# Exponent operands built on ScalarE, weight halves in other pieces, and wider moving operands in the output products of a gated attention and expert kernel

## The reference

```python
B, H, S, D = 4, 8, 768, 40
for t in range(S):                        # stabilised gated linear attention
    m_new = max(f[t] + m, i[t])
    C = exp(f[t] + m - m_new) * C + exp(i[t] - m_new) * outer(v[t], k[t])
    n = exp(f[t] + m - m_new) * n + exp(i[t] - m_new) * k[t]
    y[t] = sigmoid(o[t]) * (C @ q[t]) / max(abs(n @ q[t]), 1)
x = y.transpose(0, 2, 1, 3).reshape(3072, 320)
x = top-1 of 8 experts: gate * (relu(x @ w1[e]) @ w2[e]),  w1 320x1024, w2 1024x320
x = soft mixture with 32 slots over 8 experts (a softmax over tokens in, one over slots out)
```

## Time and profile before

| | us |
|---|---|
| median of 3 runs | 586.22 |
| lowest and highest | 584.45 and 593.98 |
| the profiled execution | 585.13 |
| its span, first to last instruction | 583.3 |
| PE busy in the span | 507.0 (87%) |
| DVE / ACT / POOL busy | 326.4 / 193.9 / 327.0 |
| mean granted TensorE clock | 0.947 |

### The profile page before, as it was taken

One profiled execution on the slowest core, in us unless ns is written; L12 is line 12 of the kernel. 1 busy time (PEld: TensorE's weight loads), 2 busy tenths in 40 slices (PEclk: granted clock), 3 DMA queues, 4 the chain that ended last, 5 costly groups with the idle time before them and its releaser, 6 DMA issues.

```text
span 583.3 us, 11329 instructions
## 1 busy us (share of the span) xinstructions
PE 507.0 (87%) x3819; PEld 429.3 (74%) x3820; DVE 326.4 (56%) x547; ACT 193.9 (33%) x424; POOL 327.0 (56%) x301
## 2 busy tenths in 40 slices
PE   0599999999993379999999999999999999979583
PEld 0388888888782368989898889889889899863222
DVE  7446687876865927435856666664654333342113
ACT  2234644646632303232323232323232323220003
POOL 2466878778775056549994959592596332102000
PEclk9999999999976569999999999999999999988897
DMA  7026898888720033456232424240411740039947
GB/s 213 0 67 226 244 310 257 275 253 268 247 85 22 0 93 102 114 147 188 104 127 87 144 82 149 71 160 11 147 67 33 248 159 6 3 110 347 319 157 270
DMA packets 30239, 86.22 MB, mean 148 GB/s; under 512 B 4720, under 2 KB 15072, under 8 KB 28160
## 3 DMA queue, kind: packets, MB, share of 16 engines
q1 hardware_dynamic: 23408, 75.07, 40.2%
q0 software_dynamic: 2480, 5.59, 3.7%
q10 hardware_dynamic: 4320, 5.15, 2.5%
HBM read 72.67 MB, written 8.37 MB: 139 GB/s over the span
## 4 chain that ended last, share of the span: by engine, by line
PE 62%; DVE 17%; issue 8%; POOL 7%; DMA 3%; ACT 1%; SPq 0%; DVEq 0%; POOLq 0%; ACTq 0%
PE bank L1335 7%; PE bank L1337 6%; PE bank L1336 6%; PE bank L1318 5%; PE bank L1320 4%; PE bank L1319 4%; PE bank L1346 4%; PE bank L1211 4%; PE bank L1194 3%; DVE ys L884 3%; PE bank L1360 3%; DVE gates L1041 3%; POOL hb L531 2%; PE bank L1464 2%; PE bank L1322 2%
## 5 line engine op out<-in xcount | busy, mean ns | idle before, releaser
L1335 PE MATMUL bank<-W_high,h_high 128*128 x248 | 79.1, 319 | 2.0 <-DVE h_low L1066 2.0
L627 POOL TENSOR_TENSOR W_high<-W,ones 128x3072 fp32r<-128x3072 f32 (+1 forms) x12 | 58.6, 4884 | 38.7 <-PE bank L1337 38.7
L1337 PE MATMUL bank<-W_low,h_high 128*128 x248 | 76.4, 308 | 0.0
L1336 PE MATMUL bank<-W_high,h_low 128*128 x248 | 76.4, 308 | 0.0
L593 POOL TENSOR_TENSOR W_low<-W,W_high 128x3072 fp32r<-128x3072 f32 (+1 forms) x12 | 74.8, 6237 | 0.9
L777 ACT ACTIVATE h_high<-bank 128x512 fp32r<-128x512 f32 x62 | 33.7, 595 | 122.9 <-PE bank L1346 118.7
L875 DVE RECIPROCAL hb<-hb 128x320 f32<-128x320 f32 x24 | 51.7, 2153 | 27.7 <-POOL hb L531 27.7
L636 POOL DMA_INDIRECT combine_slots<-gates,back_i x31 | 29.8, 961 | 60.4 <-ACT gates L765 36.1
L1022 DVE TENSOR_TENSOR yc<-bank,slot_gate 128x320 f32<-128x320 f32 x31 | 15.2, 491 | 74.9 <-PE bank L1337 74.9
L1318 PE MATMUL bank<-W_high,x_high 128*128 x124 | 52.4, 422 | 4.9 <-DVE x_high L1049 2.5
L1041 DVE TENSOR_TENSOR gates<-gates,rmx (+1 forms) x31 | 53.0, 1712 | 0.0
(11 more groups left out here) (245 smaller groups left out, 1082.3 us busy)
## 6 DMA issues: line engine op xcount, KB each, us to landing
ys<-in_kvo_rows_dram SPq DMA_DIRECT2D x24, 484.0 KB, 5.6
ys<-in_qk_columns_dram SPq DMA_DIRECT2D x24, 448.0 KB, 4.4
W<-in_moe_w_rows_dram SPq DMA_DIRECT2D x8, 1280.0 KB, 9.0
W<-in_moe_w_main_dram SPq DMA_DIRECT2D x8, 1024.0 KB, 6.4
W<-in_moe_w_rows_dram SPq DMA_DIRECT2D x10, 640.0 KB, 9.9
W<-in_moe_w_main_dram SPq DMA_DIRECT2D x10, 512.0 KB, 5.7
xs<-ys ACTq DMA_DIRECT2D x29, 160.0 KB, 2.1
W<-in_moe_w_rest_dram SPq DMA_DIRECT2D x16, 256.0 KB, 6.5
```

Source lines behind the costliest of these rows:

```text
L627: g.tensor_tensor(W_high[:, columns(e % 2, part_)], w, ones[:, 0:1].broadcast_to(list(w.shape)), ALU.mult).then_inc(high_ready, 1)
L1335: mm(dst, h_high[:, kk, :], high, start=(kk == 0), stop=False)
L1336: mm(dst, h_low[:, kk, :], high, start=False, stop=False)
L1337: last = mm(dst, h_high[:, kk, :], w2_at(W_low, slot, kk), start=False, stop=(kk == NF - 1))
```

## The change

1. `expand_gates` leaves POOL and goes to ACT. Instead of one 64x1024 and one 64x512 product per chunk there are 8 + 4 scaled copies of 64x128, four of them at the end of each of ACT's iterations 4c, 4c + 1 and 4c + 2. The signal `exp_next` comes with the last of the third four.
2. POOL's `split_low_piece` starts at i = 23 instead of 20. Pieces 0, 1 and 2 come in iterations 23, 24 and 25, and pieces 3, 4 and 5 after the loop.
3. ACT's `high_piece` has 8 pieces of 768 and 640 columns instead of 5 of 1024 and 1280, in iterations 13 to 20 instead of 17 to 21.
4. In `outputs` a product streams up to three heads (123 columns) instead of two (82). The results that are kept are the same.

```diff
@@ gpsimd
-            def expand_gates(c):
-
-                if c >= 2:
-                    pool.wait_ge(e_done, B * (c - 1))
-                pool.wait_ge(w_ready, B * (c - 1) + 1)
-                ch.step(g.tensor_tensor(exp_rows[c % 2][0:HD], split_gates[0:HD, c * P:(c + 1) * P].unsqueeze(1).broadcast_to([HD, H, P]),
-                                        head_of[0:HD, :].unsqueeze(2).broadcast_to([HD, H, P]), ALU.mult))
-                g.tensor_tensor(exp_cols[c % 2][HD:P], split_gates[HD:P, c * P:(c + 1) * P].unsqueeze(1).broadcast_to([HD, B, P]),
-                                batch_of[HD:P, :].unsqueeze(2).broadcast_to([HD, B, P]), ALU.mult).then_inc(exp_next, 1)
-                pool.wait_ge(exp_next, c)
...
-                if i < NT and b == 1 and c + 1 < C:
-                    expand_gates(c + 1)
...
-                if i >= STATES:
-                    split_low_piece(i - STATES)
+                if i >= NT - 1:
+                    split_low_piece(i - NT + 1)
+            for piece in range(3, len(LOW_PIECES)):
+                split_low_piece(piece)
@@ scalar
-            HIGH_PIECES = [(0, 0, 1024), (0, 1024, 2048), (0, 2048, W1N), (1, W1N, W1N + 1280), (1, W1N + 1280, WN)]
+            def expand_gates(c, step):
+
+                t = slice(c * P, (c + 1) * P)
+                if c >= 2 and step == 0:
+                    act.wait_ge(e_done, B * (c - 1))
+                if step < 2:
+                    for h in range(step * NP, (step + 1) * NP):
+                        s.activation(exp_rows[c % 2][0:HD, h, :], split_gates[0:HD, t], ACT.Copy, scale=head_of[0:HD, h:h + 1])
+                if step == 2:
+                    for b in range(B):
+                        last = s.activation(exp_cols[c % 2][HD:P, b, :], split_gates[HD:P, t], ACT.Copy, scale=batch_of[HD:P, b:b + 1])
+                    last.then_inc(exp_next, 1)
+
+            HIGH_PIECES = [(0, n * 768, (n + 1) * 768) for n in range(4)] + [(1, W1N + n * 640, W1N + (n + 1) * 640) for n in range(4)]
...
                 if i >= 3:
                     token_columns(i - 3)
-                if 17 <= i < 17 + len(HIGH_PIECES):
-                    high_piece(i - 17)
+                if i < NT - B and i % B < 3:
+                    expand_gates(i // B + 1, i % B)
+                if 13 <= i < 13 + len(HIGH_PIECES):
+                    high_piece(i - 13)
@@ tensor, outputs
                     for n in range(NP):
-                        mm(bank[6][:, n * 2 * DA:(n + 1) * 2 * DA], qkT[i % 3][0:QROWS, 0, n, :],
-                           blocks[b][0:QROWS, n, :, :].rearrange("p a d -> p (a d)"), start=True, stop=True)
+                        a, z = 2 * n * DA, min(2 * n + 3, H) * DA
+                        mm(bank[6][:, a:z], qkT[i % 3][0:QROWS, 0, n, :], blocks[b][0:QROWS].rearrange("p n a d -> p (n a d)")[:, a:z],
+                           start=True, stop=True)
...
-                    z = min(h + 2, H)
+                    z = min(h + 3, H)
```

## The result

| | before | changed |
|---|---|---|
| median, us | 586.07 (4 runs) | 605.74 |
| the profiled execution, us | 585.13 | 605.15 |
| its span, us | 583.3 | 603.4 |
| start of routing on DVE (`mx`), us into the span | 186.39 | 204.38 |
| last step of routing (`slot_i`), us | 204.07 | 224.95 |

The changed kernel is slower: ratio 1.031, 95% interval 1.0261 to 1.0358. One of its four executions took 850.09 us at a mean clock of 0.567; it is a disturbed run and left out of the ratio. Forecast were 606.0, with a range of 588 to 614.

What follows compares the result with a forecast made beforehand. A circle of waits between POOL and DVE was taken to bound the loop, PE in chunk 0: 585.1 - 7.4 + 14.4 + 2.5 + 0.3 - 3.0 + 13.6 = 605.5, rounded to 606 us, range 588 to 614.

Steps and rivals of the forecast that it cites:

- The new wait: PE at chunk changes waits for ACT's last four copies: 3.6 us per change, 14.4 at four changes.
- The 9.2 us step: At a chunk change, L531's step on POOL was to go from 5.6 to about 9.2 us.
- The falls of the clock: TensorE's clock falls behind PE's idle time at four chunk changes, 3.4 us each: 13.6 us, range 0 to 4 x 5.5.
- The four borders together: Chunk changes after the first: 14.4 us for waits, 13.6 for clock falls, 0.3 for ACT's copies, less 7.4 for POOL's expansion.
- The first change: From chunk 0 to 1, ACT's signal comes at 47.0 and PE, which sets the pace, loses 2.5 us.
- Chunk 0: Denser products may bring TensorE's high clock earlier there: 3.0 us gained, range 0 to 7; expansion off the path.
- 123 columns: PE's output products: weight loads set the pace and streaming lies under them, so wider products cost nothing, 0 us.
- Copies and high pieces: ACT's expansion copies fit its room; W_high pieces in iterations 13, 14, 16 to 18 overshoot: 0.3 us, range 0 to 2.5.
- Low pieces: POOL's last three pieces, after the loop under the routing, finish before its gather: nothing, or 7 us if that cover failed.
- The gap is there, the clock holds: Rival at the chunk changes: PE stands idle but its clock does not fall, 592 us, between 587 and 596; chance 0.22.
- The gap does not open: Rival in ACT's iteration 4c + 2: last four copies come out before PE needs them, 567 us; chance 0.07.
- The 7.4 us of the expansion: Taking the expansion off POOL gives back 1.85 us at each of four chunk changes, if nothing else is late.

Runs made afterwards that it cites:

- e4_filler: The changed kernel with fifteen useless 123-column products on PE ahead of its wait for the expansion at each chunk change: 591.45 us, ratio 1.0079.
- e9_high_back: The changed kernel with W_high back in 5 pieces in ACT's iterations 17 to 21: 616.07 us on a slower chip, ratio 1.0341.
- e8_earlier_low_back: The changed kernel with ACT's expansion copies one iteration earlier and POOL's low pieces back in iterations 20 to 25: 574.79 us, ratio 0.9790.
- e7_low_back: The changed kernel with POOL's low pieces back in iterations 20 to 25: 604.20 us, ratio 1.0279.
- e5_123_only: The kernel before with the 123-column output products alone: 581.12 us, ratio 0.9878.
- e6_earlier_82: The changed kernel with ACT's expansion copies one iteration earlier and output products of 82 columns: 585.73 us, ratio 0.9972.
- e0_same: The changed kernel with one more register operation per tile of gathered rows on PE's sequencer, as control: 614.81 us on a slower chip, ratio 1.0343.
- e3_act_only: The kernel before with the expansion on ACT alone, at the changed kernel's place; 82 columns, pieces as before: 616.41 us, ratio 1.0472.
- e2_pool: The changed kernel with the expansion back on POOL, the other three parts kept: 583.84 us, ratio 0.9945.
- e1_earlier: The changed kernel with ACT's expansion copies one iteration earlier, ahead of the state_ready that held them: 577.70 us, ratio 0.9815.

## Why the prediction was right, point by point

The time was right to 0.3 us and so was the mechanism, but the sum is more exact than its terms, and that is luck (its own 605.5, with the 1.1 us it names between median and profiled run, would be 606.6): against the profiled spans its terms were off by +2.4 us at the four borders, -3.5 in chunk 0 with the first change, -1.3 at the end of the loop, +2.9 in the routing and -0.8 behind it, and these cancel.

- **The new wait: right.** The signal comes from the fourth copy behind `state_ready`, PE stands 3.05 to 3.3 us (3 to 4.5 were foretold), and scores and outputs are queued behind it. e4_filler puts the wait with what follows it at 4.0 us a border, where 3.6 were summed. The 9.2 us step foretold for the border is seen only there, as 65.64 to 74.39, 8.75 us, since in the changed kernel the fall of the clock lies in the same step.
- **The falls of the clock: right, and their size nearly.** They came at all five changes, one more than was counted, and lasted about 3 to 10 us. Their price at the four later changes is 14.8 us by steps, 13.6 in the sum. The last two cost 4.3, not 3.4, and with the high pieces back (e9_high_back) all four borders take 29.4 to 29.5 us for four steps, so the 4.3 hangs on part 3. The row that priced them, 6.83 us at the low clock, has the right size for the first.
- **The four borders together** were 14.4 + 13.6 + 0.3 - 7.4 = 20.9 in the sum and measured +23.3.
- **The first change: short by the fall.** 2.5 us were summed, for the wait alone. Counted from the loop's first L531, step 4 comes after 24.4 us in the changed kernel and after 22.4 in e8_earlier_low_back, which has no wait: 2.0. With the filler it is 23.4, so the wait is 1.0 of them and the fall the rest. In e7_low_back and e9_high_back, whose low clock lasts 6.8 us there and not 3.4, it is 25.3 and 25.7, so 2.9 and 3.3 in all.
- **Chunk 0: mis-sized.** 3.0 us of gain were taken from a range of 0 to 7. Without the wait step 4 comes 6.3 us earlier (64.48 to 58.19). 0.9 of these are the loop's own start (first L531 at 36.64 and 35.75; it lies between 35.7 and 37.1 in all traces). From there to step 4 it is 27.8 us before, 23.8 in e5_123_only, so 4.0 come from the columns alone, and 22.4 in e8_earlier_low_back, 1.4 less. This rest is the expansion: leaving POOL gains nothing in chunk 0 with 82 columns (e6_earlier_82, 28.0), but is on the path with 123, once PE is at the high clock: the chain of e5_123_only has L538 and L540 in it, and its first step takes 6.96 us against 5.28. The prediction had placed it off the path there, for PE's sake, and did not ask what stays of that once PE is faster.
- **123 columns: right.** Sixteen records take 1.98 or 1.92 us at the high clock, and 3.63 at the low one, as with 82.
- **Copies and high pieces: the copies right, the pieces not.** 0.32 us a copy in the total of four (0.29 from start to start, where 0.32 was foretold). For the pieces 0.3 us were taken, for decays that come late. They cost 2.05 us in the traces (e0_same against e9_high_back, step 4 to 21), most of it in the two steps of a change with the longer low clock. The range, 0 to 2.5, holds it; the medians do not show it.
- **Low pieces: the step that failed.** "Nothing, and if that cover failed 7 us" asked only whether POOL would be done before its gather. It was, by 17 us. The cost fell on DVE, the engine of the path, whose operations with two SBUF inputs were held up by the pieces beside them: +2.9 us.
- **Left out of the sum:** the fall of the earlier trace rows at 167 is gone from the changed kernel, and from step 21 to `mx` it is 1.3 us shorter. The late low pieces are not needed for that, nor is the earlier high clock: e3_act_only has neither and takes the same 18.08 us, as do e7_low_back and e8_earlier_low_back (18.08, 18.07) with the low pieces in their old place. What these three share is the expansion off POOL. With it on POOL, e5_123_only still falls, for 3.4 us, and takes 18.35; e2_pool, with the pieces of both kinds moved, does not (18.07). The idle times of PE ahead of that place are 1.25 and 1.28 us in these two, so it is a near thing, and each is one profiled execution.

**The rivals.** "The gap is there, the clock holds" was forecast at 592 and is what e4_filler built: 591.45, with the same terms off and cancelling. "The gap does not open" was forecast at 567 and is what e1_earlier and e8_earlier_low_back built: 577.7 and 574.8. The 7.4 us of the expansion come back only in part. From step 4 to step 21 e8_earlier_low_back saves 102.55 - 96.58 = 6.0 us. Its chain shows why, here at the change from chunk 2 to 3:

```profile
105.22 1.75 PE bank L1202 x16
106.98 0.68 PE bank L1213 x16
107.66 0.48 PE bank L1219 x3
108.14 0.47 PE bank L1172 x2
108.60 1.12 PE bank L1184 x16
109.72 1.05 PE bank L1196 x8
110.77 1.75 PE bank L1202 x16
112.52 0.79 PE bank L1235 x24
```

There is no L531 in it. Once POOL's circle has no expansion, PE's own work bounds most of the loop, with 5.5 us a step and 0.79 for the router in each chunk; from 143 on the chain has L531 in it again. So e8_earlier_low_back stands 7.8 us over the 567: 1.4 for this, 0.7 in chunk 0 (6.3 where 7 were taken), 2.1 at the end of the loop (1.3 where 3.4 were taken), and 3.5 behind `slot_i` (382.7 us, against 379.2), which is in that stretch's own spread.

The Trainium skill (TensorE: Matmul & The Clock Gate, "HAM oscillation — how this bites in real kernels") has the price paid at every burst behind an idle time. The trace agrees with five falls at five idle times of 3.05 to 3.3 us, and e4_filler with none when the idle time is filled. The page's case is a wait for a DMA; here PE waited for another engine.

What stays open: how part 3 lengthens the low clock at the last two changes (6.8 us at 69 and 99, 10.2 at 126 and 157), since PE's idle time ahead of them is nearly the same with it and without (3.11 and 3.18 us, 3.04 and 3.31). In the three kernels that have it the clock fell there 1.0 to 1.3 us before PE went on, in e9_high_back at most 0.7 us before; but e3_act_only, without part 3 and with 82 columns, has 10.2 us or more at each of its four falls and does not fit this. What of its length is due to the columns is open too.

## What to carry to other kernels

Work that leaves a busy engine needs a place on the new one that is ahead of that engine's own late waits: against the same parts with the expansion on POOL (e2_pool, 0.9945), the twelve copies cost 3.7% behind `state_ready` and gave 1.3% one iteration earlier. With 82 columns they cost 4.7% and gave 0.3% (e3_act_only, e6_earlier_82), and the interval of the latter includes no change at all. Price a new wait on TensorE twice, once for the standstill (here 4.0 us with what follows it) and once for the clock that falls behind it (3.1 to 4.3 us), and remember that filler products remove the second but not the first. When work is moved to where its own engine is idle, look at the operands of whoever is on the path beside it, since the two may share a way into SBUF. The fastest version found here is e8_earlier_low_back, 574.79 us: the changed kernel with the copies one iteration earlier and the low pieces back.

## What the runs showed of the hardware

- Two DVE operations of 192 columns with both inputs in SBUF took 2.19 and 1.42 us beside POOL's 128x1024 subtraction, and 0.36 and 0.35 without it. The engine counts as busy meanwhile, so the loss stands in no list of waits.
- Streaming 123 columns in place of 82 cost no time at either clock (3.63 us for sixteen records at the low one, 1.98 at the high one) and brought the high clock earlier in chunk 0: the first fast group starts at 38.20 in place of 55.21.
- A scaled copy of 64x128 in SBUF on ScalarE is recorded with 381 ns; in a row of four the next starts 0.29 us later, and the four take 1.27 us.
- In the changed kernel TensorE's clock fell at each of the five idle times of 3.05 to 3.3 us, and came back within 3.4 to 10.2 us. Idle times of 1.0 to 1.5 us went either way: the clock fell up to 1.5 us after PE had gone on, at 166.9, 162.9 and 52.6 (the kernel before, e5_123_only, e1_earlier), and held in e2_pool behind 1.5 us at 46 and 1.28 at 160.
